# Twelve slots for ranks and list, the first expert named by the last fills, a gather of row 0 ahead, choice behind the tokens

## Chip, core and metric

The kernel runs on one core of a Trainium2 chip. The metric is the device time of one execution in microseconds. The engines are TensorE (PE), VectorE (DVE), ScalarE (ACT), GpSimd (POOL) and SyncE (SP, which issues DMAs).

## What is computed

```python
# linear attention with decay: B 4, H 8, S 768, D 48
state = alpha[t] * state + k[t] (outer) v[t];  y[t] = q[t] @ state
x = y as [3072 tokens, 384]
# first layer: 8 experts of 384 tokens each, F 1024
logits = x @ w_gate                     # [3072, 8]
for idx in argsort(-logits.flatten()):  # highest first
    tok, e = idx // 8, idx % 8
    if assigned[tok] < 0 and counts[e] < 384: assigned[tok] = e; counts[e] += 1
out[mask_e] = relu(x[mask_e] @ w1[e]) @ w2[e]
# second layer, the same weights for all tokens, G 1536
out = (silu(x @ w_gate2) * (x @ w_val)) @ w_out
```

## The kernel before

The attention part works through 24 units (4 batches by 6 chunks of 128 tokens), writes its rows to x_rows in memory and leaves the logits as [128 partitions, 24 tiles, 8 experts]; token t * 128 + p is in tile t, partition p. Its last units overlap the start of the routing.

The greedy assignment is computed in phases: in each, all free tokens choose their best open expert, and a search finds the threshold at which the first expert is full. The first phase has four rounds (first_rounds_vector, first_rounds_tensor). In each, DVE compares every token's best logit with 31 cuts (compare, L809), PE counts by cut and expert (L840), DVE marks the full cuts (find_full, L816 and L817), PE counts those (L844) and DVE raises the base (raise_base, L822). Then `take` (L954 to L968) gives tokens above the base to their experts; PE sums them (ps_room, L1011); DVE finds the newly full expert (L887, L888), marks its tokens (L891, L894), and writes the expert's number to `order` (tell_order, L944 and L946), for which SP waits before it loads that expert's weights. PE ranks the marked tokens within their tile and sums the tiles (L1015 and L1016, 24 columns each). DVE turns the ranks into rows and columns of the list (L900 to L914), builds at_row, one 128 x 128 matrix for each of 24 tiles in two halves (L922), PE multiplies 24 times (L1023), and DVE reduces the sums to slot_token (L928), which has 3 x 128 token numbers. GpSimd gathers the three tiles of rows (gather_first, L1615). PE turns each with three transposes (L1877), ACT and DVE split it in x_high and x_low (L1683, L1686; L1761, L1764), and the first expert's products begin (L1778). While GpSimd gathers, PE runs 20 products of 512 columns that nothing reads (WARM_TURNS, L1871).

Each expert is then computed for its 384 tokens: 8 stages of up and down products with a ring of four weight chunks, 12 stages of gate, value and output products; every product is done in three parts, from a high and a low part of both operands. A group of nine products is one stage of one of these. The seven experts but the last carry the next phase's routing between their stages: `route` puts one step of vector_step and tensor_step behind each stage. Step 10 (s == take + 2) names and marks, step 11 ranks, 12 and 13 build at_row, 14 reduces and settles, 15 chooses. The rank products are issued after stage 2 of the second layer, the list products after stage 5. ACT makes w_high from w_raw, and w_low is made by GpSimd in the loop and by DVE (L1749) for the first four chunks. The choice of the second phase (choose, L980 to L989) stands behind these on DVE and ahead of x_low.

Each link of the routing waits on its own semaphore count for the one before; the order of all work on an engine is the order in which it is written. If a check of the routing fails, an exact routing and a second run of the layers follow.

Of the kernel before, what the change touches and what calls it, by code (L numbers as in the profile page):

```python
# [32 lines left out]
WARM_TURNS = 20  # L33
# [510 lines left out]
SLOTS = 10  # L544

# [4 lines left out]
QUICK_LINKS = 48  # L550
# [5 lines left out]
Operands = namedtuple("Operands", "best is_over got room_now newly_full rank past past_next at_col cols_past row")  # L556
# [14 lines left out]
class QuickRouting:  # L571
# [22 lines left out]
    def __init__(self, nc, ctx, logits, slot_token, order, failed):  # L594
# [3 lines left out]
        def sem(name):  # L598
# [19 lines left out]
        self.cut_tab = sb("cut_tab", [P, ROUNDS, CUTS - 1])  # L618
        self.cuts = sb("cuts", [P, ROUNDS, CUTS - 1])
# [10 lines left out]
        self.place = rest[:, TILES * E:TILES * (E + 1)]  # L630
        self.lows = sb("lows", [P, B, CH - 1])
# [12 lines left out]
        self.mine = sb("mine", [P, TILES], BF16)  # L644
        self.before = sb("before", [P, TILES])
        rank = sb("rank", [P, TILES])
        past = sb("past", [P, TILES, 2 * T3])
        at_col = sb("at_col", [P, TILES, T3])
        cols_past = sb("cols_past", [P, TILES])
        row = sb("row", [P, TILES], BF16)  # L650
        self.token_parts = sb("token_parts", [P, TILES, T3, 2], BF16)
        self.still_free = sb("still_free", [P, TILES], BF16)
        self.first = Operands(self.best, is_over, got, room_now, newly_full, rank, past[:, :, 0:T3], past[:, :, T3:2 * T3], at_col,
                              cols_past, row)
# [5 lines left out]
        self.below = sb("below", [P, P], BF16)  # L660
# [3 lines left out]
        self.col_starts = sb("col_starts", [P, T3 + 1])  # L664
        self.lane = sb("lane", [P, 1])
        self.tiles = sb("tiles", [P, TILES])
# [22 lines left out]
        self.judged = sem("judged")  # L689
        self.at = [0, 0]  # L690


    CONSTS = 5
    SET = 12 + FINE_ROUNDS

    def use(self, bank):
# [4 lines left out]
        self.ps_rank = bank[:, 4 * E:4 * E + 2 * TILES]  # L701
        self.ps_token = bank[:, 4 * E + 2 * TILES:4 * E + 2 * TILES + 2 * T3]
# [5 lines left out]
        def words(count):  # L708
# [9 lines left out]
        past_next, at_col = (shared[:, n * TILES * T3:(n + 1) * TILES * T3].rearrange("p (t c) -> p t c", t=TILES)  # L718
                             for n in range(2))

        assert at[0] > CAP
        best, self.low_apart, self.expert_numbers = (words(count) for count in (TILES, 1, E))
        self.later = Operands(best, self.free, got, room_now, newly_full, self.free, self.first.past, past_next, at_col,
                              self.first.cols_past, self.number)

    def load(self, sp, consts):
        for dst, name in ((self.cut_tab[:, :, :].rearrange("p a b -> p (a b)"), "cuts"),
                          (self.numbers[:], "count"),
                          (self.col_starts[:], "col_starts"), (self.lane[:], "lane"), (self.tiles[:], "tiles")):
            sp.dma_start(dst, consts[name]).then_inc(self.consts_in, 16)  # L730

    def set_up(self, pool):
        for ap, value in ((self.ones, 1.0), (self.ones2, 1.0), (self.assigned, 0.0), (self.free_cap, BIG),
                          (self.room, float(CAP)), (self.room_or_big, float(CAP)),
                          (self.full_before, 0.0), (self.zeros, 0.0), (self.filled, 0.0), (self.odd, 0.0)):
            pool.memset(ap[:], value).then_inc(self.ready, 1)
        for n in range(FINE_ROUNDS):
            pool.memset(self.fine_scale[:, n:n + 1], float(FINE_CUTS) ** -(n + 1)).then_inc(self.ready, 1)

    def set_up_tables(self, pool):  # L740
        pool.wait_ge(self.consts_in, 16 * self.CONSTS)

        pool.tensor_scalar(self.below[:], self.numbers[:], self.lane[:, 0:1], -1.0, ALU.is_lt,
                           ALU.mult).then_inc(self.ready, 1)
# [80 lines left out]
    def first_rounds_vector(self, dve):  # L825
        for n in range(ROUNDS):
            if n > 0:
                self.raise_base(dve, n, self.cuts[:, n - 1, 0:1])
            for i in range(2):
                tiles = slice(i * TILES // 2, (i + 1) * TILES // 2)  # L830
                self.compare(dve, self.best[:, tiles], tiles, self.cuts[:, n, :])
            self.find_full(dve, n + 1, CUTS - 1)
        self.raise_base(dve, ROUNDS, self.cuts[:, ROUNDS - 1, 0:1])

    def first_rounds_tensor(self, pe):
        for n in range(ROUNDS):
            for i in range(2):
                pe.wait_ge(self.over_cut_ready, 2 * n + i + 1)
                for t in range(i * TILES // 2, (i + 1) * TILES // 2):
                    mm = pe.matmul(self.ps_count[0:CUTS - 1, :], self.at_row[:, t, 0:CUTS - 1], self.choice[:, t, :],  # L840
# [3 lines left out]
            pe.matmul(self.ps_full, self.cut_full[0:CUTS - 1, 0:1].broadcast_to([CUTS - 1, P]),  # L844
                      self.ones[0:CUTS - 1, 0:1], start=True, stop=True).then_inc(self.cut_found, 1)
# [5 lines left out]
    def vector_step(self, dve, p, s):  # L851

        link = lambda ins: self.link(dve, ins)
        o = self.operands(p)
# [29 lines left out]
        if s == take + 2:  # L884

            dve.wait_ge(self.got_summed, p + 1)
            link(dve.tensor_tensor(o.room_now[:, :], self.room[:], self.ps_room, ALU.subtract))  # L887
            link(dve.scalar_tensor_tensor(out=o.newly_full[:, :], in0=o.room_now[:, :], scalar=0.5,  # L888
                                          in1=self.full_before[:], op0=ALU.is_lt, op1=ALU.subtract))
            newly_full = o.newly_full[:, :].unsqueeze(1).broadcast_to(te)  # L890
            link(dve.tensor_tensor(self.marks[:], self.assigned[:], newly_full, ALU.mult))  # L891
            if o is self.later:
                self.tell_order(dve, p, o)
            dve.tensor_reduce(self.mine[:], self.marks[:], AX_X, ALU.max).then_inc(self.mine_ready, 1)  # L894
            if o is self.first:
                self.tell_order(dve, p, o)
        if s == take + 3:

            dve.wait_ge(self.mine_ranked, p + 1)
            link(dve.tensor_tensor_scan(self.before[:], self.ps_rank[:, TILES:2 * TILES], self.zeros[:], 0.0,  # L900
                                        ALU.add, ALU.add))
            link(dve.tensor_tensor(o.rank[:, :], self.ps_rank[:, 0:TILES], self.before[:], ALU.add))
            link(dve.tensor_tensor(o.rank[:, :], o.rank[:, :], self.mine[:], ALU.mult))
            tc = [P, TILES, T3]
            for past, c in ((o.past, 0), (o.past_next, 1)):
                link(dve.tensor_tensor(past, o.rank[:, :].unsqueeze(2).broadcast_to(tc),
                                       self.col_starts[:, c:c + T3].unsqueeze(1).broadcast_to(tc), ALU.is_ge))
            link(dve.tensor_tensor(o.at_col[:, :, :], o.past, o.past_next, ALU.subtract))
            link(dve.tensor_tensor(o.cols_past[:, :], o.past[:, :, 1], o.past_next[:, :, 1], ALU.add))
            link(dve.scalar_tensor_tensor(out=o.row[:, :], in0=o.cols_past[:, :], scalar=-float(P),  # L910
                                          in1=o.rank[:, :], op0=ALU.mult, op1=ALU.add))

            link(dve.tensor_scalar(self.token_parts[:, :, :, 0], o.at_col[:, :, :], self.lane[:, 0:1], None, ALU.mult))
# [1076 lines left out]
```

## Time and profile before

| | |
|---|---|
| median of 3 runs | 849.14 us (849.04 to 849.73) |
| profiled execution | 849.57 us, span 847.7 us |
| PE busy | 819.5 us |
| DVE busy | 508.6 us |
| ACT, POOL busy | 299.5, 236.1 us |

Times in the rows are microseconds from the start of the span. A row of the chain gives start, length and what the end of the program was waiting for at that time; a row of a timeline gives start, length, engine, line, operation, tiles and shapes, and in brackets how long the engine had been idle and what ended it.

### The profile page before, as it was taken

Reading aid. Unit: us, or ns where it says so; the run is one execution under the profiler, and the core shown is the slowest. Engines: PE = TensorE matmul, PEld = TensorE weight load, DVE = VectorE, ACT = ScalarE, POOL = GpSimd, SP = SyncE. Lnnn points to the kernel's source line nnn. Section 1 sums busy time; section 2 is a strip of 40 time slices with the busy share of each in tenths; the row PEclk is TensorE's granted clock in tenths of the full one; section 3 lists DMA queues with packets and bytes.
Section 4 is the critical chain, followed back from the end, with each engine's and each line's share of the span. In section 5 each row is a group of like instructions: output and inputs, shape, how many; then the busy total and the mean of one; then the engine's idle time right before and its main releaser. Section 6 shows DMA issues by size and latency. Waiting matters only on the chain.

```text
span 847.7 us, 16569 instructions
## 1 busy us (share of the span) xinstructions
PE 819.5 (97%) x6116; PEld 783.7 (92%) x6116; DVE 508.6 (60%) x1095; ACT 299.5 (35%) x607; POOL 236.1 (28%) x263
## 2 busy tenths in 40 slices
PE   9999993899999999999999999999999999999995
PEld 5889883699999999999999999999999999999995
DVE  9999986846554655465546554665466546642332
ACT  2566652432343224323332333233323332333221
POOL 4222210388613041304130414050405040504001
PEclk9999996899999999999999999999999999999998
DMA  8898852402300230023002300230023002300000
GB/s 294 282 323 290 285 173 73 161 1 75 103 19 9 74 102 19 9 74 102 19 9 74 102 19 9 74 102 19 9 74 102 19 9 74 102 18 11 1 1 32
DMA packets 25858, 70.98 MB, mean 84 GB/s; under 512 B 3808, under 2 KB 10464, under 8 KB 25824
## 3 DMA queue, kind: packets, MB, share of 16 engines
q1 hardware_dynamic: 19296, 56.39, 20.2%
q0 software_dynamic: 3072, 9.44, 3.3%
q10 hardware_dynamic: 3456, 4.72, 1.5%
q8 instruction: 18, 0.29, 0.1%
q14 instruction: 16, 0.13, 0.1%
HBM read 61.10 MB, written 9.44 MB: 83 GB/s over the span
## 4 chain that ended last, share of the span: by engine, by line
PE 81%; DVE 2%; issue 1%; DMA 0%; POOL 0%; POOLq 0%; ACT 0%; ACTq 0%
PE ps_up L1778 48%; PE ps_acc L1778 30%; PE ps_turn_again L1002 1%; PE ps_turn_again L1023 1%; PE ps_turn L1784 1%; PE ps_turn_again L840 0%; DVE quick_at_row L922 0%; DMA x_tok<-x_rows,slot_token 0%; DVE quick_at_row L809 0%; PE ps_up L1784 0%; POOL x_tok L1615 0%; POOLq L1911 0%; DVE quick_base L822 0%; PE ps_turn_again L844 0%; DVE quick_fills L816 0%
## 5 line engine op out<-in xcount | busy, mean ns | idle before, releaser
L1778 PE MATMUL ps_up<-z_high,gated_high 128*128 128x384 f32 x576 | 197.8, 343 | 0.0
L1778 PE MATMUL ps_up<-z_high,gated_low 128*128 128x384 f32 x576 | 194.6, 338 | 0.0
L1778 PE MATMUL ps_up<-z_low,gated_high 128*128 128x384 f32 x576 | 193.6, 336 | 0.0
L1560 POOL TENSOR_TENSOR w_low<-w_raw,w_high 128x384 fp32r<-128x384 f32 x120 | 118.6, 1014 | 248.3 <-ACT w_high L1641 248.0
L1778 PEld LDWEIGHTS ps_up<-z_high,gated_high 128*128 128x128 f32 x576 | 108.3, 188 | 0.0
L1778 PEld LDWEIGHTS ps_up<-z_low,gated_high 128*128 128x128 f32 x576 | 108.1, 188 | 0.2
L1778 PEld LDWEIGHTS ps_up<-z_high,gated_low 128*128 128x128 f32 x576 | 108.3, 188 | 0.0
L1725 DVE TENSOR_TENSOR act_out<-ps_up,act_out 128x384 f32<-128x384 f32 x96 | 53.4, 557 | 89.8 <-ACT act_out L1657 88.1
L1660 ACT CAST u_high<-ps_up 128x384 fp32r<-128x384 f32 x96 | 46.1, 480 | 169.3 <-DVE ps_up L1729 169.3
L1657 ACT ACTIVATE act_out<-ps_up 128x384 f32<-128x384 f32 x96 | 47.2, 492 | 142.0 <-PE ps_up L1778 141.9
L1778 PE MATMUL ps_acc<-gated_high,u_high 128*128 128x384 f32 x288 | 97.4, 338 | 0.0
L1778 PE MATMUL ps_acc<-gated_low,u_high 128*128 128x384 f32 x288 | 96.8, 336 | 0.0
L1778 PE MATMUL ps_acc<-gated_high,u_low 128*128 128x384 f32 x288 | 96.5, 335 | 0.0
L1583 POOL DMA_INDIRECT out<-o_tok,to_rows x24 | 23.6, 985 | 224.5 <-ACT o_tok L1669 189.9
L1732 DVE TENSOR_TENSOR u_low<-ps_up,u_high 128x384 fp32r<-128x384 f32 x96 | 53.6, 558 | 52.4 <-ACT u_high L1660 51.9
L1714 DVE SCALAR_TENSOR_TENSOR h_low<-ps_up,h_high 128x384 fp32r<-128x384 f32 x64 | 35.7, 558 | 71.0 <-ACT h_high L1637 69.2
L1729 DVE TENSOR_TENSOR ps_up<-act_out,ps_up 128x384 f32<-128x384 f32 x96 | 54.0, 562 | 39.5 <-PE ps_up L1778 37.3
L1641 ACT CAST w_high<-w_raw 128x768 fp32r<-128x768 f32 x64 | 53.6, 837 | 47.6 <-PE ps_acc L1778 34.9
L1778 PE MATMUL ps_up<-x_high,w_high 128*128 128x384 f32 x192 | 66.8, 348 | 0.1
L1778 PE MATMUL ps_acc<-h_high,w_high 128*128 128x384 f32 x192 | 64.8, 337 | 0.0
L1778 PE MATMUL ps_up<-x_low,w_high 128*128 128x384 f32 x192 | 64.4, 336 | 0.0
L1778 PE MATMUL ps_up<-x_high,w_low 128*128 128x384 f32 x192 | 64.4, 336 | 0.0
(220 smaller groups left out, 1420.9 us busy)
## 6 DMA issues: line engine op xcount, KB each, us to landing
w_raw<-in_experts SPq DMA_DIRECT2D x64, 384.0 KB, 3.0
qka_in<-in_qka SPq DMA_DIRECT2D x22, 770.5 KB, 5.8
gated_raw<-in_gated SPq DMA_DIRECT2D x12, 576.0 KB, 5.7
v_in<-in_v SPq DMA_DIRECT2D x24, 192.0 KB, 5.0
x_rows<-y_rows ACTq DMA_DIRECT2D x24, 192.0 KB, 3.7
qka_in<-in_qka SPq DMA_DIRECT2D x2, 512.0 KB, 5.1
qka_in<-in_qka SPq DMA_DIRECT2D x2, 258.5 KB, 3.8
out<-o_tok,to_rows POOLq DMA_INDIRECT x24
```

The source lines that it names most:

```text
L1002: mm = pe.matmul(self.ps_count, self.at_row[:, j, :], self.slot_choice[:, j, :], start=(j == 0), stop=(j == SLOTS - 1))
L1023: mm = pe.matmul(self.ps_token, self.at_row[:, t, :], self.token_parts[:, t, :, :].rearrange("p a c -> p (a c)"), start=(t == 0), stop=(t ...
L1560: part = pool.tensor_tensor(w.low[:, m % RING, cols], w.raw[:, m % RING, cols], w.high[:, m % RING, cols].bitcast(F32), ALU.subtract)
L1583: pool.indirect_dma_start(out=out, out_offset=bass.IndirectOffsetOnAxis(ap=to_rows[:, t:t + 1], axis=0), in_=o_tok[:, t, :], in_offset=Non ...
L1641: act.copy(w.high[:, m % RING, :], w.raw[:, m % RING, :]).then_inc(w_high_ready, 1)
L1657: act.activation(act_out[:, j % 2, :], ps_up[j % 2][0][:, 0:CAP], ACT.Sigmoid).then_inc(sigm_ready, 1)
L1660: act.copy(u_high[:, j % 2, :], ps_up[j % 2][0][:, 0:CAP]).then_inc(u_high_ready, 1)
L1714: dve.scalar_tensor_tensor(out=h_low[:, m % 2, :], in0=ps_up[m % 2][0][:, 0:CAP], scalar=0.0, in1=h_high[:, m % 2, :].bitcast(F32), op0=AL ...
L1725: dve.tensor_tensor(act_out[:, j % 2, :], ps_up[j % 2][0][:, 0:CAP], act_out[:, j % 2, :], ALU.mult).then_inc(silu_ready, 1)
L1729: dve.tensor_tensor(ps_up[j % 2][0][:, 0:CAP], act_out[:, j % 2, :], ps_up[j % 2][1][:, 0:CAP], ALU.mult).then_inc(gated_ready, 1)
L1732: dve.tensor_tensor(u_low[:, j % 2, :], ps_up[j % 2][0][:, 0:CAP], u_high[:, j % 2, :].bitcast(F32), ALU.subtract).then_inc(u_low_ready, 1)
L1778: mm = pe.matmul(acc, lhs[a], rhs[b], start=(first and i == 0), stop=(last and i == 2))
```

## The change

The list has 12 slots a partition instead of 24 tiles: a token's slot is its place among the marked tokens of its partition (place_mine), and hold_mine finds the tile of each slot. PE ranks partitions with one product of one column (ahead, mine_count) where it had two of 24, and the list takes 12 products with at_row of 12 x 128. A partition with more than 12 marked tokens sets the failure flag through `most`.

In the first phase the fourth round has 32 cuts, and its fills go as [32, 8] straight to PE, which sums them per expert; the expert with the highest sum is the first. The take, the room and settling come behind the list on DVE (first_settle_vector), and PE's room product behind its list products. GpSimd folds the expert's number to `order` with five small operations (tell_first). Before them it issues one gather of row 0, 128 times, into x_tok. Of the first four w_low, two are made on DVE and two on GpSimd, behind the gathers. The warm products are 6, 4 and 3, ahead of the transposes of the three tiles. choose stands behind x_low. A tensor of 96 words and the changed sizes move the addresses of what is allocated later.

```diff
-WARM_TURNS = 20
+WARM_TURNS = (6, 4, 3)
+LISTED = 12
+SPACER = 96
+FIRST_LOWS = 2
@@ first_rounds_vector, behind the last compare
-            self.find_full(dve, n + 1, CUTS - 1)
-        self.raise_base(dve, ROUNDS, self.cuts[:, ROUNDS - 1, 0:1])
+            if n < ROUNDS - 1:
+                self.find_full(dve, n + 1, CUTS - 1)
+        link(dve.tensor_tensor(self.base_under[:], self.base[:], self.cuts[:, ROUNDS - 1, 1:2], ALU.subtract))
+        dve.wait_ge(self.cuts_counted, ROUNDS)
+        dve.tensor_tensor(self.last_fills[:, :], self.ps_count[0:CUTS, :], self.room_or_big[0:CUTS, :],
+                          ALU.is_ge).then_inc(self.cut_full_ready, 1)
+        dve.wait_ge(self.cut_found, ROUNDS)
+        link(dve.tensor_reduce(self.level[:], self.ps_room, AX_X, ALU.max))
+        dve.tensor_tensor(o.newly_full[:, :], self.ps_room, self.level[:, 0:1].broadcast_to([P, E]),
+                          ALU.is_equal).then_inc(self.first_known, 1)
+        link(dve.scalar_tensor_tensor(out=self.base[:], in0=self.level[:], ...))
+        link(dve.tensor_tensor(self.marks[:], self.choice[:], o.newly_full ...))
+        link(dve.tensor_reduce(self.mine_any[:], self.marks[:], AX_X, ALU.max))
+        link(dve.scalar_tensor_tensor(out=o.mine[:, :], in0=self.best[:], scalar=self.base[:, 0:1], in1=self.mine_any[:],
+                                      op0=ALU.is_ge, op1=ALU.mult))
+    def first_list_vector(self, dve):
+        self.count_mine(dve, o.mine[:, :])
+        self.place_mine(dve, 0, o)
+        self.hold_mine(dve, o)
+        dve.wait_ge(self.mine_ranked, 1)
+        self.rank_mine(dve, o)
+        self.part_tokens(dve, o)
+        for i in range(2):
+            self.find_rows(dve, o, i)
+        self.list_tokens(dve, 0)
+    def tell_first(self, pool):
+        pool.wait_ge(self.first_known, 1)
+        pool.tensor_tensor(self.first_part[:], self.first.newly_full[0:1, :], self.tiles[0:1, 0:E], ALU.mult)...
+        for n, half in enumerate((4, 2, 1)):
+            pool.tensor_tensor(self.first_part[:, 0:half], self.first_part[:, 0:half], self.first_part[:, half:2 * half], ALU.add)...
+        pool.tensor_scalar(self.order[0:1, 0:1], self.first_part[:, 0:1], float(E - 1), None, ALU.min)...
+    def first_settle_vector(self, dve):
+        self.take(dve, 0)
+        self.leave_room(dve, 0, o)
+        self.settle(dve, 0, o)
+    def first_list_tensor(self, pe):
+        self.rank_tensor(pe, 0)
+        self.list_tensor(pe, 0, 1)
+        self.room_tensor(pe, 0)
+    def place_mine(self, dve, p, o):
+        link(dve.tensor_tensor_scan(self.mine_place, o.mine[:, :], self.zeros[:], 0.0, ALU.add, ALU.add))
+        link(dve.tensor_tensor(o.place_of[:, :], self.mine_place, o.mine[:, :], ALU.mult))
+    def hold_mine(self, dve, o):      # by_slot = [P, 12, 24]
+        link(dve.tensor_tensor(self.mine_held, place_of, slot numbers, ALU.is_equal))
+        link(dve.tensor_tensor(self.mine_part, self.mine_held, tile numbers, ALU.mult))
+        link(dve.tensor_reduce(self.slot_tile[:], self.mine_part, AX_X, ALU.add))
+    def rank_mine(self, dve, o):      # five links of 12 elements: slot_rank, rank, past_one, cols_past, row
+    def part_tokens(self, dve, o):    # three links of 36: at_col, token_parts 0, token_parts 1
@@ tensor_step, s == take + 5
-                for t in range(i * TILES // 2, (i + 1) * TILES // 2):
-                    mm = pe.matmul(self.ps_token, self.at_row[:, t, :],
+            for j in range(i * LISTED // 2, (i + 1) * LISTED // 2):
+                mm = pe.matmul(self.ps_token, self.at_row[:, j, :], ...
@@ gather_first
+                pool.indirect_dma_start(
+                    out=x_tok[:, 0, :], out_offset=None, in_=x_rows,
+                    in_offset=bass.IndirectOffsetOnAxis(ap=quick.row_zero[:, 0:1], axis=0)).then_inc(quick.warmed, 16)
+                quick.tell_first(pool)
+                pool.wait_ge(quick.warmed, 16)
                 pool.wait_ge(quick.listed, 1)
                 for t in range(T3):
                     pool.indirect_dma_start(
...
+                for m in range(FIRST_LOWS, RING):
+                    pool.wait_ge(w_low_ready, m)
+                    split_low(0, m)
@@ vector, not again
+                quick.first_rounds_vector(dve)
+                quick.first_list_vector(dve)
+                quick.first_settle_vector(dve)
+                quick.keep_apart(dve)
+                for m in range(FIRST_LOWS):
+                    first_low(m)
                 for t in range(T3 - 1):
                     dve.wait_ge(first_high_ready, t + 1)
...
+                quick.choose(dve)
+                quick.end_first_phase()
@@ tensor, not again
                 quick.first_rounds_tensor(pe)
-                for s in range(quick.TAKE, steps):
-                    route(0, s, False)
-                for n in range(WARM_TURNS):
-                    pe.matmul(ps_up[0][0] ...)
+                quick.first_list_tensor(pe)
                 for t in range(T3):
+                    for n in range(WARM_TURNS[t]):
+                        pe.matmul(ps_up[0][0] ...)
                     pe.wait_ge(first_rows[t], 16)
```

## Rows read from the trace of the kernel before

**Rows 1.** The page, busy time, share and instructions of each engine.
```profile
PE 819.5 (97%) x6116; PEld 783.7 (92%) x6116; DVE 508.6 (60%) x1095; ACT 299.5 (35%) x607; POOL 236.1 (28%) x263
```

**Rows 2.** The chain of waits, 141 to 164 us: start, length, what.
```profile
141.11 0.17 DVE quick_fills L816
...
147.53 3.44 DVE quick_at_row L922 x2
...
151.54 0.18 DVE slot_token L928
...
156.45 3.04 DMA x_tok<-x_rows,slot_token
...
159.53 0.34 PE ps_acc L1877
...
160.21 3.39 PE ps_up L1778 x18
163.60 1.56 PE ps_acc L1778 x9
```

**Rows 3.** The timeline of DVE, 142 to 165 us.
```profile
142.64 0.49 DVE L959 TENSOR_REDUCE quick_got_rows<-quick_got 128x8 bf16<-128x192 bf16 x1
...
143.74 0.17 DVE L888 SCALAR_TENSOR_TENSOR quick_newly_full<-quick_room_now,quick_full_before 128x8 f32<-128x8 f32 x1
143.94 0.36 DVE L891 TENSOR_TENSOR quick_marks<-quick_assigned,quick_newly_full 128x192 bf16<-128x192 bf16 x1
...
152.62 3.56 DVE L1749 TENSOR_TENSOR w_low<-w_raw,w_high 128x768 fp32r<-128x768 f32 x4
...
156.50 0.35 DVE L980 TENSOR_TENSOR quick_limited<-logits,ps_turn_again 128x192 f32<-128x192 f32 x1
...
158.84 0.16 DVE L989 COPY quick_base<-ps_turn_again 128x1 f32<-128x1 f32 x1
...
160.40 0.48 DVE L1764 TENSOR_TENSOR x_low<-ps_up,x_high 128x128 fp32r<-128x128 f32 x2
...
163.76 0.41 DVE L864 TENSOR_TENSOR quick_at_row<-ps_turn_again,quick_numbers 128x240 f32<-128x240 f32 x1
```

**Rows 4.** The timeline of PE, 151 to 164 us.
```profile
151.36 6.87 PE L1871 MATMUL ps_up<-quick_idt 128*128 128x512 bf16 x20
158.06 0.82 PE L1877 MATMUL ps_acc<-quick_idt,x_tok 128*128 128x128 f32 x6
...
163.79 0.33 PE L1778 MATMUL ps_acc<-h_low,w_high 128*128 128x384 f32 x1
```

**Rows 5.** POOL: the first gathers, a copy, and all gathers of the loop (min/median/max).
```profile
152.69 1.94 POOL L1615 DMA_INDIRECT x_tok<-x_rows,slot_token  x1 [35.44 <-DVE slot_token L928]
154.93 1.21 POOL L1615 DMA_INDIRECT x_tok<-x_rows,slot_token  x1 [0.30 <-issue]
...
219.85 0.18 POOL L1547 COPY from_rows<-slot_token 128x3 uint32<-128x3 uint32 x1 [0.28 <-DVE slot_token L928]
...
L1552 POOL DMA_INDIRECT x_tok<-x_rows,from_rows x21: 942/957/1007, 220.8 to 735.9; - x21
```

**Rows 6.** Windows: length, busy of PE, PEld, DVE, ACT, POOL, granted clock, DMA.
```profile
132.00:134.00 2.00, 1.14 (x25) 0.89 (x25) 1.15 (x4) 1.89 (x2) 0.00 (x0) 0.58 0.24 68
...
156.00:156.25 0.25, 0.25 (x2) 0.15 (x1) 0.25 (x2) 0.00 (x0) 0.15 (x1) 0.54 0.44 172
```

**Rows 7.** The chain of waits in the loop's first turn, 288 to 305 us.
```profile
288.12 1.56 PE ps_acc L1778 x9
289.69 0.03 PE ps_turn_again L1015
...
304.00 0.60 PE ps_turn_again L1023 x24
304.60 3.26 PE ps_up L1778 x18
```

**Rows 8.** The timeline of ACT, the first cast of the first expert's weights.
```profile
149.31 1.78 ACT L1641 CAST w_high<-w_raw 128x768 fp32r<-128x768 f32 x2 [11.38 <-DMA w_raw<-in_experts]
```

More of the change, by code:

```diff
@@ L555 @@
 Programs = namedtuple("Programs", "sync gpsimd scalar vector tensor")
-Operands = namedtuple("Operands", "best is_over got room_now newly_full rank past past_next at_col cols_past row")
+Operands = namedtuple("Operands", "best is_over got room_now newly_full mine place_of rank row at_col")
 def has_failed(eng, quick):
@@ L643, in __init__ @@
         self.marks = sb("marks", te, BF16)
[L644 to L654, printed above, removed]
+        self.mine_count = sb("mine_count", [P, 1], BF16)
+        self.most = sb("most", [P, PHASES + 1])
+        self.mine_any = sb("mine_any", [P, TILES])
+        mine = sb("mine", [P, TILES])
+        place_of = sb("place_of", [P, TILES])
+        self.slot_tile = sb("slot_tile", [P, LISTED])
+        self.slot_rank = sb("slot_rank", [P, LISTED])
+        self.past_one = sb("past_one", [P, LISTED])
+        self.cols_past = sb("cols_past", [P, LISTED])
+        rank = sb("rank", [P, LISTED])
+        row = sb("row", [P, LISTED], BF16)
+        at_col = sb("at_col", [P, LISTED, T3])
+        self.token_parts = sb("token_parts", [P, LISTED, T3, 2], BF16)
+        self.still_free = sb("still_free", [P, TILES + PHASES + 1], BF16)
+        self.any_wrong = sb("any_wrong", [P, 1], BF16)
+        self.first = Operands(self.best, is_over, got, room_now, newly_full, mine, place_of, rank, row, at_col)
         self.odd = sb("odd", [P, 3])
@@ L843, in first_rounds_tensor @@
             pe.wait_ge(self.cut_full_ready, n + 1)
[L844 to L845 removed]
+            if last:
+                mm = pe.matmul(self.ps_room, self.ones[0:CUTS, :], self.last_fills[:, :], start=True, stop=True)
+            else:
+                mm = pe.matmul(self.ps_full, self.cut_full[0:CUTS - 1, 0:1].broadcast_to([CUTS - 1, P]),
+                               self.ones[0:CUTS - 1, 0:1], start=True, stop=True)
@@ L853, in vector_step @@
         link = lambda ins: self.link(dve, ins)
-        o = self.operands(p)
+        o = self.later
         te = [P, TILES, E]
@@ L892, in vector_step @@
[L892 to L896, printed above, removed]
+            link(dve.tensor_tensor(self.marks[:], self.assigned[:],
+                                   o.newly_full[:, :].unsqueeze(1).broadcast_to(te), ALU.mult))
+            self.tell_order(dve, p, o)
+            link(dve.tensor_reduce(o.mine[:, :], self.marks[:], AX_X, ALU.max))
@@ L897, in vector_step @@
+            self.place_mine(dve, p, o)
+            self.count_mine(dve, o.mine[:, :])
         if s == take + 3:
             dve.wait_ge(self.mine_ranked, p + 1)
[L900 to L911, printed above, removed]
@@ L925, in vector_step @@
[L925 to L938 removed]
+            self.hold_mine(dve, o)
@@ L939, in vector_step @@
+            self.rank_mine(dve, o)
+        if s == take + 4:
+            self.part_tokens(dve, o)
+        if s in (take + 4, take + 5):
+            self.find_rows(dve, o, s - take - 4)
+        if s == take + 6:
+            self.list_tokens(dve, p)
+            self.settle(dve, p, o)
         if s == take + 7:
@@ L1740, in expert, with first_low @@
                 dve.tensor_copy(o_tok[:, T3 - 1, :], ps_acc[T3 - 1][:, 0:DM]).then_inc(last_o_copied, 1)
-            if not again:
-                quick.first_rounds_vector(dve)
-                quick.take(dve, 0)
-                for s in range(quick.TAKE + 1, steps - 1):
-                    route(0, s, False)
-            for m in range(RING):
+            def first_low(m):
                 dve.wait_ge(w_high_ready, m + 1)
@@ L1750, in vector @@
                                   ALU.subtract).then_inc(w_low_ready, 1)
-            if not again:
-                quick.keep_apart(dve)
-                quick.choose(dve)
-                quick.end_first_phase()
             if again:
+                for m in range(RING):
+                    first_low(m)
                 for k in range(K1):
```

197 lines of the change are left out of this document (130 added, 67 removed).

## The prediction

> **What bounds the kernel now.** I read the page's engine totals first: PE is busy for 97% of the span [rows 1]. Then the chain of waits in order of time. After the attention part it leaves PE and runs mostly through DVE until 151.7 us, then through GpSimd and its gathers to 159.5, and from 160.21 on it is PE without a break until the tail [rows 2]. From there to the end each PE microsecond taken out is one off the time, and DVE or GpSimd work counts only if PE waits for it. Ahead of 160.21 it is the other way round: DVE's links count, and PE only with what it does after the list. So the sum has two parts: the entry (when the first expert's first product starts) and the seven later routing phases, as they stand in PE's queue.
>
> **The list of the first expert.** I take start-to-start times on DVE as the price of a link: about 0.20 us for 24 elements or fewer (L888 at 143.74, L891 at 143.94), 0.39 for 192 and 0.44 for 240 (a busy time of 0.36 and 0.41 and 0.03 to the next; [rows 3]). From the end of the last L816 at 141.28 to the start of the token reduction at 151.54 are 10.26 us [rows 2]. After the change the same stretch is: PE's 32-row product as L844's, 0.27 with its hand-overs; level, newly_full and base 0.62; marks and mine_any 0.78; mine, count, scan, place 0.84; three operations on 12 x 24 = 288 elements, which the trace does not have: not under the 240-element link (0.44) and not over it in proportion (0.44 x 1.2 = 0.53), taken 0.49, 1.47 together; five links of rank_mine 1.00; three of part_tokens on 36 elements, between 0.20 and 0.39, near the small one, 0.23 each, 0.69; at_row with 768 instead of 1536 elements per half, (1.72 - 0.12) / 2 + 0.12, about 0.89, twice, 1.78; the last six products instead of twelve 0.32. Sum 7.77, so 2.5 us earlier: the reduction starts at about 149.1. Gone from the path are cut_full, the take (0.27 + 0.39 + 0.49 + 0.39) and leave_room, which come later on DVE. The rank product is issued after count_mine and hides behind scan, place and hold (2 us against 0.25). The bounds of this step are 2.1 to 2.8.
>
> **The gathers.** Before, the first issue took 1.94 us and the second 1.21; the 21 of the loop take 0.957 in the middle, 1.007 at most [rows 5]. If the extra is that of a first use, the gather of row 0 pays it around 135 us, when GpSimd has nothing else and stores have landed, and the real ones save 0.94 + 0.26 = 1.2 us. If they save nothing it is 0; the row of the loop is the nearest for a second use, so 1.2. Third issue then at about 152.65, and with its 3.04 us to landing [rows 2] the last rows are there at 155.7 instead of 159.49; the first at 153.1, the second at 154.4.
>
> Beside the two long issues DVE ran L1749, whose operands are both in SBUF; the third, from 156.45, lay beside choose [rows 2, 3, 5]. The Trainium skill (SBUF — State Buffer, "SBUF: two separate sides") says that a VectorE operation with two SBUF inputs and a GpSimd operation that reads SBUF take one shared port by turns, each for a whole instruction. By that rule the excess comes from the neighbour, not from first use; the third issue would then lie beside the moved first_low and take up to 1.94 again, its rows landing at 156.7. The trace can't tell the two apart; it only shows that L1749 itself was not slowed. That is a rival below.
>
> **PE up to the first product.** PE's queue holds the room product between list and warm turns, and it waits for the take: list at 149.1, then 0.2 and 1.15 for is_over, got, got_rows [rows 3], so 150.5. The turns therefore start at 150.55, against 151.36 before [rows 4]. The granted clock fell to 0.50 in 132 to 134 and went back to 1.00 at 156.2 [rows 6], so 1.2 GHz until then, 2.4 after; PE had been busy without a gap for 4.87 us when it rose. A turn is 0.427 at 1.2 GHz (the twenty: 4.87 / 0.427 = 11.4 of them, then 8.6 x 0.216). Now: six turns to 153.1; three transposes at twice the 0.11 pitch of [rows 4] to 153.8; four turns to 155.5; the clock, if it again takes 4.87 us from 150.55, rises at 155.4; three transposes 0.33, three turns 0.65, to 156.45; last transposes and cast as before 0.68 (159.53 to 160.21), first product at 157.1. That is 3.1 us earlier than 160.21. Two ends: a clock that is up by 154.5 leaves only the rows, 155.7 + 0.68 = 156.4, 3.8 earlier; one that isn't up at all gives 158.4, 1.8 earlier, with what then follows in the rival. So of the 3.7 us by which list and gather move, about 0.6 goes to turns put between the transposes.
>
> **What is late next.** (a) choose (L980 to L989, 2.5 us [rows 3]) now stands behind x_low. x_low ended 0.67 us after the first product; then choose to +3.2, h_low to +3.8. PE took h_low's first product at 163.79, 3.58 after 160.21 [rows 2, 4]. So a wait of 0.2 us, 0 to 0.5; the next h_low has over a microsecond of room. (b) Weights: DVE does take, leave_room, settle and keep_apart from 149.3 to about 152.7, then two w_low at 0.89 each to 154.4, before PE needs them. The other two, by GpSimd, take 2 us each, behind the third issue and w_low 1, to 156.4 and 158.4; PE needs them 5 and 8 us after 157.1. Without that room each would cost its lateness. Casts of w_high began at 149.31 [rows 8], soon enough even if the first order came no earlier. (c) The five small GpSimd operations that tell SP the expert: the copy of 3 numbers took 0.18 [rows 5], so 0.9 to 1.5 in all from 141.95; even 3 us would put the order no later than before, where it came after the whole take, and by (b) no cast would be late. GpSimd's queue behind them holds only the gather, which waits for 149.3 anyway. (d) Two memsets more, one table load less and lane_part lie in GpSimd's idle time in attention, 0.1 us at worst.
>
> **The seven later phases.** PE's list products fall from 24 to 12: 0.60 us for 24 [rows 7], so 0.30 a phase; of the two rank products (0.03 and 0.02) one goes, 0.03. 7 x 0.33 = 2.3 us, all on the path, bounds 2.0 to 2.5. DVE gets 0.6 us more in step 10 and about the same in step 11 (2.5 against 2.5), and less in 12 and 13. PE has no wait for DVE in this stretch now: it runs on after the 24 products into the next stage [rows 7], and the longest step now, choose with 2.5 us, is hidden in stages 4.8 us long (from the rank products at 289.69 to the list products at 304.00 are three). So nothing.
>
> **Sum.** -3.1 + 0.2 - 2.3 = -5.2 us. The profiled execution took 849.57 (span 847.7 and 1.9 around it), which is 0.43 over the median of 849.14. From the first the sum gives 844.4, from the second 843.9; I say 844.1.
>
> **Rivals.**
> 1. The clock stays low past the first product. For it: in the new entry PE's work is cut by waits and turns, and short bursts of 1 us or so from 133 to 149 raised nothing. If it takes 4.87 us from the first product at 158.4, the products up to then lose half, 2.4 us: the entry is 0.6 later than before plus 0.2, the phases give 2.3, so 847.7. If it rises at 158, 845.4. Against: the turns begin earlier than before and join with gaps near 0.
> 2. The port, as above: a third issue of up to 1.94 instead of 0.957 puts the last rows at 156.7, the first product at 157.4: 844.4 from the median, and with a first issue of 1.94 too 845.3. What speaks for it is that both long issues lay beside L1749.
> 3. Slower: other addresses. All big operands move in SBUF. PE spends 1.56 us on nine products (173.6 ns each, more than 384 columns at 2.4 GHz need), and the kernel has 468 x 8 = 3744 of them. From 1.4 ns a product (0.8%) this eats the 5.2 us; at 1% it is 6.5 us and the time 850.4. Against: the products of h with the ring's weights at 163.60 [rows 2] and of the gated weights with u at 288.12 [rows 7] come from quite different places and both take 1.56 for nine.
> 4. It doesn't do what it says: were more than 12 tokens of an expert in one partition, the list would be short and the kernel would route and compute again, eight stretches of 85 us more. Counting the reference's own assignment, no partition has more than 9.
>
> **Chances.** The forecast's own course (842.9 to 845.1) 0.62; rivals 1 and 2 beyond that (845.1 to 847.7) 0.26; rival 3 0.11 (0.07 slower, 0.03 within 0.2%, 0.01 still faster); rival 4 0.01. The far end of rival 1 is within 0.2% too, 0.01. Of a measurement of this kernel about 0.2%, 1.7 us, can be told from no change. Faster 0.88, same 0.04, slower 0.08. The range is 842.7 to 846.9: below, everything at its good end (3.8, 0 wait, 2.5: 842.8); above, most of rival 1.
>
> **What would show it.** The first expert's token reduction near 149.1; three issues of about 1.0, 0.95, 0.95; the clock's rise before 157; the first product at 156.4 to 158.4; one PE wait of about 0.2 us for h_low; 0.30 for the list products of each phase; the nine-product groups still 1.56. It is wrong if the loop groups differ from 1.56, if a PE wait recurs in each phase, or if the rise comes after the first product.

## The result, and the profile after

The changed kernel takes 841.19 us (median of 4 runs, 840.79 to 841.45); the kernel before took 849.28 beside it. The ratio is 0.9902 with a 95% interval of 0.9890 to 0.9914: faster by 8.1 us, where I forecast 5.2 and a time of 844.1. The direction was right, the size was not, and the time lies below the range (842.7 to 846.9). The profiled execution took 841.45.

The page after, answering to [rows 1]:

```profile
span 839.5 us, 16444 instructions
...
PE 811.9 (97%) x6005; PEld 776.7 (93%) x6005; DVE 505.7 (60%) x1134; ACT 299.8 (36%) x607; POOL 242.9 (29%) x276
```

PE is 7.6 us less busy. Eight lists at 0.30 less are 2.4, and the warm turns (6.87 before, 2.72 + 1.91 + 0.81 after) are 1.4 less; the other half must come from products that both kernels have. The chain of waits of the kernel after over the entry, answering to [rows 2] (start, length, what):

```profile
141.23 0.17 DVE quick_last_fills L862
...
147.17 1.84 DVE quick_at_row L980 x2
...
149.42 0.17 DVE slot_token L987
...
150.39 3.19 DMA x_tok<-x_rows,slot_token
...
157.66 0.67 DVE x_low L1903 x3
158.34 0.27 DVE quick_limited L1106
...
160.59 0.17 DVE quick_base L1115
160.98 0.57 DVE h_low L1853
161.59 1.51 PE ps_acc L1919 x7
```

The list reduction starts at 149.42 (forecast 149.1), and h_low has become a link of the chain, behind choose, as forecast. PE's timeline, answering to [rows 4], has the first product at 157.67 (forecast 157.1), and in brackets the idle time ahead of h_low's first product:

```profile
150.75 2.72 PE L2012 MATMUL ps_up<-quick_idt 128*128 128x512 bf16 x6
...
157.67 0.44 PE L1919 MATMUL ps_up<-x_high,w_high 128*128 128x384 f32 x1
...
161.59 0.44 PE L1919 MATMUL ps_acc<-h_low,w_high 128*128 128x384 f32 x1 [0.16 <-DVE h_low L1853]
```

GpSimd's timeline, answering to [rows 5]. The third issue takes 1.64:

```profile
133.69 1.19 POOL L1744 DMA_INDIRECT x_tok<-x_rows,quick_row_zero  x1 [16.43 <-DMA x_rows<-y_rows]
...
143.34 0.23 POOL L900 TENSOR_SCALAR order<-quick_first_part 1x1 int32<-1x1 f32 x1
...
150.39 1.06 POOL L1751 DMA_INDIRECT x_tok<-x_rows,slot_token  x1 [6.82 <-DVE slot_token L987]
151.75 0.95 POOL L1751 DMA_INDIRECT x_tok<-x_rows,slot_token  x1 [0.30 <-issue]
153.01 1.64 POOL L1751 DMA_INDIRECT x_tok<-x_rows,slot_token  x1 [0.30 <-issue]
```

Entry and phases together can't give 8.1. The rest is found by holding the same point of two turns of the loop side by side, the count products of choose, which stand behind the same stage in each. The chain of the kernel before, then of the kernel after:

```profile
245.68 3.13 PE ps_up L1778 x18
...
256.61 0.25 PE ps_turn_again L1002 x10
...
294.56 3.16 PE ps_up L1778 x18
...
341.81 0.25 PE ps_turn_again L1002 x10
```

```profile
253.73 0.25 PE ps_turn_again L1128 x10
...
289.87 1.56 PE ps_acc L1919 x9
291.43 3.12 PE ps_up L1919 x18
...
300.80 0.30 PE ps_turn_again L1154 x12
...
338.14 0.25 PE ps_turn_again L1128 x10
```

A turn takes 341.81 - 256.61 = 85.20 before and 338.14 - 253.73 = 84.41 after, 0.79 less, of which list and rank explain 0.33. The rest is in the groups of eighteen: the gate and value products of one stage take 3.12 us instead of 3.16. Twelve such stages in a turn make 12 x 0.04 = 0.48. The nine-product groups stay at 1.56. So the eighteen had been running at 1.58 for nine, and I had compared only the nines. The row at 245.68 is a group of eighteen of the other kind, up products of x with the ring's weights: of the same shape and in the same execution, they take 3.13.

### The profile page after: what moved, and what is told of

Read it like the earlier page. It is cut to its first block, busy times and chain, and to the rows that moved or that the text cites. A ratio compares the mean times of both kernels' runs of the same rounds, so it can differ in the third digit from the quotient of the medians.

```text
span 839.5 us, 16444 instructions
## 1 busy us (share of the span) xinstructions
PE 811.9 (97%) x6005; PEld 776.7 (93%) x6005; DVE 505.7 (60%) x1134; ACT 299.8 (36%) x607; POOL 242.9 (29%) x276
## 4 chain that ended last, share of the span: by engine, by line
PE 81%; DVE 2%; issue 1%; DMA 0%; POOLq 0%; ACT 0%; POOL 0%; DVEq 0%; ACTq 0%
PE ps_up L1919 48%; PE ps_acc L1919 30%; PE ps_turn_again L1128 1%; PE ps_turn L1925 1%; PE ps_turn_again L917 0%; DMA x_tok<-x_rows,slot_token 0%; DVE quick_at_row L831 0%; PE ps_turn_again L1154 0%; PE ps_up L1925 0%; DVE quick_at_row L980 0%; PE ps_up L2012 0%; POOLq L2051 0%; PE ps_acc L2017 0%; DVE quick_base L844 0%; DVE x_low L1903 0%
## 5 line engine op out<-in xcount | busy, mean ns | idle before, releaser
L1919 PE MATMUL ps_up<-z_high,gated_high 128*128 128x384 f32 x576 | 195.7, 340 | 0.0
L1691 POOL TENSOR_TENSOR w_low<-w_raw,w_high 128x384 fp32r<-128x384 f32 x124 | 122.3, 1013 | 243.6 <-ACT w_high L1780 243.1
L1919 PE MATMUL ps_up<-z_high,gated_low 128*128 128x384 f32 x576 | 192.5, 334 | 0.0
L1919 PE MATMUL ps_acc<-h_low,w_high 128*128 128x384 f32 x192 | 64.4, 336 | 0.2 <-DVE h_low L1853 0.2
```

Of the source, the lines that this page charges most:

```text
L1691: part = pool.tensor_tensor(w.low[:, m % RING, cols], w.raw[:, m % RING, cols], w.high[:, m % RING, cols].bitcast(F32), ALU.subtract)
L1919: mm = pe.matmul(acc, lhs[a], rhs[b], start=(first and i == 0), stop=(last and i == 2))
```

## The experiments

All medians are in us. "Before" is the kernel before, run beside it on the same chip.

| kernel | median | before | ratio (95%) |
|---|---|---|---|
| e1_before_all32 | 845.92 | 849.42 | 0.9955 (0.9940 to 0.9969) |
| e2_after_back32 | 845.39 | 849.42 | 0.9952 (0.9935 to 0.9968) |
| e4_before_z32 | 848.94 | 849.42 | 0.9998 (0.9989 to 1.0008) |
| e3_after_no_row0 | 840.33 | 849.42 | 0.9892 (0.9875 to 0.9908) |
| e5_before_all32_z64 | 846.67 | 849.38 | 0.9961 (0.9947 to 0.9975) |
| e7_before_all64 | 849.66 | 849.38 | 1.0004 (0.9994 to 1.0013) |
| e8_before_gated_high32_all64 | 845.92 | 849.38 | 0.9953 (0.9936 to 0.9970) |
| e9_no_row0_choose_split | 840.15 | 849.38 | 0.9886 (0.9869 to 0.9902) |
| e10_after_no_turns | 842.63 | 849.30 | 0.9918 (0.9901 to 0.9934) |
| e11_after_turns_631 | 841.06 | 849.30 | 0.9900 (0.9883 to 0.9916) |
| e12_before_choose_first | 849.19 | 849.30 | 0.9999 (0.9989 to 1.0008) |
| e13_no_row0_split_631 | 840.19 | 849.30 | 0.9889 (0.9872 to 0.9905) |

### The addresses

In the kernel before, the tensors of the layers lie at byte addresses (in a partition) with rest 0 by 64 (what is left over when the address is divided by 64), all but gated_high, which is allocated earlier and has rest 32. The change moves all the others by 32 more than a multiple of 64: they have rest 32 too. (I reckoned the addresses from the sizes of all that is allocated, each start rounded up to 32 bytes; no trace shows them.) The first pair makes this move alone, in each direction.

```diff
 e1, before, behind the tensors of the routing
+        sb("pad", [P, 8])
 e2, after
-SPACER = 96
+SPACER = 88
```

> The kernel before with 8 words of unused memory ahead of all that the layers allocate: gated_low, the ring, x, h, z, u, act_out and the rest lie exactly where the changed kernel has them, nothing else changes. Theory A (the addresses made the products of z with the gated weights shorter, 3.12 instead of 3.16 us for eighteen, some 3.7 us in all): 845.5 us, eighteen products in 3.12, first product still at 160.2. Rival B (the new routing steps in the phases, with other DVE and GpSimd work beside PE, made the products shorter): 849.2, 3.16. Rival C (the trace's 0.04 is noise of one execution): 849.2.

> The changed kernel with its spacer of 88 words instead of 96: all layer tensors lie where the kernel before has them. Theory A: 3.7 us longer than the changed kernel, 844.9 us, eighteen products of z in 3.16. This would be the time of the change without its addresses, and is near the 844.1 that was forecast. Rivals B and C: 841.2, 3.12.

Padding alone, with no other change, takes 849.42 - 845.92 = 3.5 us off the kernel before; taking the move back costs the kernel after 845.39 - 841.19 = 4.2. A group of eighteen in the chain of e1, then a group of e2:

```profile
295.47 3.12 PE ps_up L1779 x18
```

```profile
193.02 3.17 PE ps_up L1919 x18
```

96 stages (8 experts by 12) times 0.04 is 3.8, between the two. This part of the gain is shown from both sides, though e1's median is uncertain by some tenths: its five runs lie at 845.34 to 845.92 and at 846.88 and 846.95, and the profiled one, 846.95, lost time to a clock that fell (last section). What is left open is which operand's place does it. e4 moves z and all behind it, and so leaves gated_low where it was; e5 moves all and z and u back to rest 0; e7 moves by 64 instead of 32; e8 moves gated_high too, to rest 0.

```diff
 e4, before, ahead of z_high
+        sb("pad_z", [P, 8])
 e5: the pads of e1 and e4
 e7: the pad of e1 with 16 words
 e8: the pad of e1, and ahead of gated_high
+        sb("pad_g", [P, 8], F32)
```

> The kernel before with 8 unused words right ahead of z_high: z, u, act_out, o_tok move by 32 bytes; gated_low, the ring, x and h stay. If A holds and it is the place of the streamed operand z by itself, or of z against gated_high, that counts: 845.5, like all moved. If it is the place of gated_low (the stationary operand, against gated_high), 849.2.

> The kernel before with 8 unused words ahead of gated_low and 8 more ahead of z_high: gated_low, the ring, x and h are at +32 bytes, z, u, act_out, o_tok at +64. Moving everything by 32 gave 845.9, moving z and what follows by 32 alone gave 848.9. Theory G (only gated_low's place against gated_high's counts): 845.9 again. Theory R (stationary and streamed operand must leave the same rest when the address is divided by 64; gated_high lies at 32, z would be back at 0): slow again, 849.

> The kernel before with 16 unused words ahead of gated_low: all that the layers allocate moves by 64 bytes, so every rest by 64 is as before. Theory R: 849.4, eighteen products of z in 3.16. If any other place than the old one would do: 845.9.

> The kernel before with 8 unused words ahead of gated_high and 8 ahead of gated_low: gated_high moves from a rest of 32 to one of 0, the layers' tensors move by 64 and keep their rest of 0, so weights and streamed operands have one rest, 0, where the fast kernels have 32. Theory R: 845.9, 3.12. If the layers' own rest of 32 is what counts: 849.4, 3.16.

The chains of e5, e7 and e8, one fence each (e4 has 3.15 for its group at 294.48):

```profile
294.10 3.12 PE ps_up L1780 x18
297.21 1.58 PE ps_acc L1780 x9
```

```profile
294.79 3.17 PE ps_up L1779 x18
```

```profile
294.58 3.12 PE ps_up L1780 x18
```

The column "turn" is one turn of the loop, from one of its count products to the same one a turn later.

| kernel | gated_high, gated_low, z by 64 | eighteen | turn | time |
|---|---|---|---|---|
| before | 32, 0, 0 | 3.16 | 85.20 | 849.3 |
| e7 | 32, 0, 0 (all 64 on) | 3.17 | 85.21 | 849.66 |
| e4 | 32, 0, 32 | 3.15 | 85.13 | 848.94 |
| e5 | 32, 32, 0 | 3.12 | 84.87 | 846.67 |
| e1 | 32, 32, 32 | 3.12 | 84.75 | 845.92 |
| e8 | 0, 0, 0 | 3.12 | 84.70 | 845.92 |

The eighteen are slow when gated_high and gated_low have unlike rests and fast when they have the same, 32 or 0. The turns of the loop say the same, and the clock of the entry has no part in them. A move of 64 does nothing, one of z alone 0.01 a group. In this group PE loads them in turn (high, low, high for the three parts of a product) and streams z; the up and down products load w_high and w_low in turn, which have like rests in both kernels and took 1.56 for nine in both. e8 rules out that 32 is simply the better rest. e5 rules out the other rule on trial, that the loaded and the streamed operand must agree: z is at 0 and the gated weights at 32, and the eighteen take 3.12. Whether 64 is the number that counts is not shown: where the two have like rests by 64 here, they have like rests by 128 and by 256 too. A second, smaller effect is in e5: u at 0 with both gated weights at 32 lengthens the group of nine with u (1.58), and e5 takes 0.75 us more than e1. In that group PE loads u and streams the gated weights. I have no rule for that one, since with gated_high at 32, gated_low at 0 and u at 0 (before) this group takes 1.56. Why the engine's loads or reads care for the rest, no run here shows.

### The gather of row 0 and the third issue

```diff
 e3, after, gather_first
-                pool.indirect_dma_start(
-                    out=x_tok[:, 0, :], out_offset=None, in_=x_rows,
-                    in_offset=bass.IndirectOffsetOnAxis(ap=quick.row_zero[:, 0:1], axis=0)).then_inc(quick.warmed, 16)
...
-                pool.wait_ge(quick.warmed, 16)
```

> The changed kernel without the gather of row 0. If the long first issues of before (1.94 and 1.21 us) were a first use of the gather, as the forecast had it: first issue again about 1.9, second 1.2, the rows 1.2 us later, first product at about 158.6 instead of 157.67, time 842.0. If they were the port shared with L1749 on DVE, whose operands are both in memory: first and second issue stay at 1.0 to 1.2 beside the small DVE operations, third 1.64 beside the two w_low as now, time 841.2 to 841.4.

GpSimd, DVE and PE of e3, from three timelines:

```profile
149.75 1.30 POOL L1747 DMA_INDIRECT x_tok<-x_rows,slot_token  x1 [6.33 <-DVE slot_token L987]
151.36 0.96 POOL L1747 DMA_INDIRECT x_tok<-x_rows,slot_token  x1 [0.31 <-issue]
152.63 0.95 POOL L1747 DMA_INDIRECT x_tok<-x_rows,slot_token  x1 [0.30 <-ACT w_high L1776]
...
152.74 1.83 DVE L1879 TENSOR_TENSOR w_low<-w_raw,w_high 128x768 fp32r<-128x768 f32 x2
...
156.72 0.45 PE L1915 MATMUL ps_up<-x_high,w_high 128*128 128x384 f32 x1
```

Neither course that I expected came: without the gather of row 0 the kernel is faster still, 841.19 to 840.33, and the first product moves from 157.67 to 156.72. The list reduction starts at 149.28 here and the first issue 0.47 behind it; with row 0 gathered it starts 0.97 behind (149.42, 150.39), while its own length falls only from 1.30 to 1.06. So the row-0 gather, with the wait for it, costs 0.26 net on the first issue, and through that start another 0.69 on the third. What sets this delay is open: in the kernel before, with no gather ahead, the first issue comes 1.15 behind the start of the reduction (151.54, 152.69). The kernel after has w_low beginning at 152.87, ahead of the third issue:

```profile
152.87 1.82 DVE L1883 TENSOR_TENSOR w_low<-w_raw,w_high 128x768 fp32r<-128x768 f32 x2
```

It starts 0.14 before the issue (153.01, 1.64 long). In e3 the issue is first by 0.11 and takes 0.95 (e9 and e13 likewise). e2, whose third issue is again behind its w_low, shows the same price (e10 and e11 too, 1.65 and 1.64):

```profile
152.93 1.65 POOL L1751 DMA_INDIRECT x_tok<-x_rows,slot_token  x1 [0.30 <-ACT w_high L1780]
```

The reverse test is on the kernel before: take w_low away from beside the issues, leave the first use.

```diff
 e12, before, vector
+            if not again:
+                quick.keep_apart(dve)
+                quick.choose(dve)
+                quick.end_first_phase()
             for m in range(RING):
                 dve.wait_ge(w_high_ready, m + 1)
                 dve.tensor_tensor(w.low[:, m, :], ...)
-            if not again:
-                quick.keep_apart(dve)
-                quick.choose(dve)
-                quick.end_first_phase()
```

> The kernel before with keep_apart and choose ahead of the four w_low (L1749) instead of behind them. Port theory (the gather's issue is long where it starts beside a DVE operation with both operands in memory): the first two issues, now beside settle and choose, take 1.0 to 1.3 and 0.95 us instead of 1.94 and 1.21, and one that starts during a w_low takes 1.2 to 1.9. First-use theory: 1.94 and 1.21 as before. The w_low end at about 159.1, so the time may stay near 849.

The gathers and w_low of e12:

```profile
152.66 1.17 POOL L1615 DMA_INDIRECT x_tok<-x_rows,slot_token  x1 [35.45 <-DVE slot_token L928]
154.14 0.96 POOL L1615 DMA_INDIRECT x_tok<-x_rows,slot_token  x1 [0.30 <-issue]
155.40 0.95 POOL L1615 DMA_INDIRECT x_tok<-x_rows,slot_token  x1 [0.30 <-issue]
...
155.54 3.56 DVE L1753 TENSOR_TENSOR w_low<-w_raw,w_high 128x768 fp32r<-128x768 f32 x4
```

The issues of 1.94 and 1.21 in [rows 5] become 1.17 and 0.96: most of the excess was the neighbour. The 0.22 that are left (0.35 in e3) may be a first use or the small DVE operations beside it; no run parts the two. Each w_low lasts 0.95 by its own record in the kernels before and after. In the kernel after the one that was under way at the third issue's start ends at 153.83, and the issue ends 0.82 behind it (154.65); in the kernel before, at the second issue, the two ends are 155.32 and 156.14, 0.82 apart. So, as far as these two rows show, the issue waits for the end of that operation and is not held by the next. This agrees with the port rule of the Trainium skill (SBUF — State Buffer, "SBUF: two separate sides"), by which the operation that starts first has the shared port for the whole instruction. The other half of the rule, that whatever comes second is blocked, the traces don't bear out for DVE: in e3 and e12 w_low starts second, within the third issue, and lasts 0.95 all the same. The time of e12 is no other (849.19): its rows come earlier, but the twenty turns start at 151.48 and hold PE until 158.35, and DVE's x_low, now behind the four w_low, keeps PE's next products until 160.50.

### The wait for h_low and the turns

e9 is e3 with the first four operations of choose between the x_low of tile 0 and of tile 1; e13 is e9 with WARM_TURNS (6, 3, 1); e11 and e10 change only the turns of the kernel after.

```diff
 e9 and e13, without row 0, vector, in the loop over tiles
+                    if t == 0:
+                        quick.choose(dve, both=False)
...
-                quick.choose(dve)
+                quick.choose_cuts(dve)
 e11 and e13
-WARM_TURNS = (6, 4, 3)
+WARM_TURNS = (6, 3, 1)
 e10
+WARM_TURNS = (0, 0, 0)
```

> The changed kernel without the gather of row 0 (840.33) and with the first four links of choose put between the first two x_low, where DVE waited for ACT for 0.9 to 1.5 us; the last four stay behind x_low. Theory: the wait for the first h_low goes (PE's first product of h_low at 3.6 instead of 3.9 us after the first product), 0.3 us: 840.0. Rival: the four links, 1.3 us, delay the second x_low instead and with it the first product, since DVE's gap was 0.88 us without the row-0 gather: 840.3 to 840.7.

> The changed kernel without the gather of row 0, with choose split around the second x_low, and 6, 3 and 1 warm products: what the runs so far point to. If the turns between the transposes still cost: 839.6. If the rows or DVE bound it: 840.1, as without the shorter turns.

> The changed kernel with 6, 3 and 1 warm products instead of 6, 4 and 3. If the three last transposes are late because of the turns between (the first product at 157.67, the rows at about 156.1), the first product comes 0.5 to 0.9 us earlier and the time is 840.5. If the third rows bound it, 841.0 to 841.2.

> The changed kernel without any of its 13 warm products. The transposes then start when the rows land, so the first product at about 156.9 instead of 157.67, in PE time that is at 1.2 GHz. The forecast's reckoning (the clock rises 4.9 us after PE begins to be busy without a gap, whenever that is): rise at about 161.8, the products up to then at half speed, 2.4 us lost, 842.8 us in all. Rival (the rise comes at a time that the program's start sets, about 155 to 157 us, if only PE is then busy; it was 156.1 to 156.3 in both first traces, with the turns starting 0.6 us apart): here PE is idle before the rows, so the rise comes at the next such time, 158.5 to 163: 841.5 to 843.5. Neither expects less than 841.2.

PE's first product and the first of h_low in e9:

```profile
157.09 0.44 PE L1924 MATMUL ps_up<-x_high,w_high 128*128 128x384 f32 x1
...
160.69 0.33 PE L1924 MATMUL ps_acc<-h_low,w_high 128*128 128x384 f32 x1
```

160.69 - 157.09 = 3.60, as in the kernel before (3.58), so the wait is gone; but the first product is 0.37 later than in e3, because the second x_low is (156.59 against 156.16). 840.15 against 840.33 is within the spread of the two (839.89 to 840.66). e13, with fewer turns, is at 840.19: its first product comes at 156.67, but then PE waits 0.19 for x_low. e11 (841.06) equals the kernel after (841.19): its third tile of rows comes no earlier, and PE stands idle for it 1.22 us. Its timeline:

```profile
156.99 0.33 PE L2017 MATMUL ps_acc<-quick_idt,x_tok 128*128 128x128 f32 x1 [1.22 <-DMA x_tok<-x_rows,slot_token]
```

So in the kernel after the rows are as late as the turns; taking turns away gains nothing while the third issue is blocked. Without any turns (e10) the first product comes at the same time (157.72) and the clock later. Windows of e10 (length, busy of PE, PEld, DVE, ACT, POOL, granted clock, DMA):

```profile
158.00:160.00 2.00, 2.00 (x7) 2.00 (x8) 1.83 (x8) 1.37 (x2) 0.81 (x1) 0.50 0.91 277
160.00:161.00 1.00, 1.00 (x5) 1.00 (x4) 0.76 (x3) 0.00 (x0) 0.00 (x0) 0.50 0.98 283
161.00:161.25 0.25, 0.25 (x2) 0.25 (x2) 0.00 (x0) 0.25 (x1) 0.00 (x0) 0.50 1.23 283
161.25:161.50 0.25, 0.25 (x3) 0.25 (x2) 0.00 (x0) 0.24 (x1) 0.00 (x0) 1.00 0.64 258
```

The clock is 0.50 until 161.25 and 1.00 behind it, so 3.5 us of products run at half speed. That is 1.8 us lost, less the 0.3 for h_low, which is then hidden: 1.5, and 842.63 - 841.19 = 1.44 is what the thirteen turns are worth.

## Why the prediction was wrong

**The sum.** Of the 8.1 us, 2.2 come from the entry (the first product of h_low moved from 163.79 to 161.59), 2.3 from the phases (7 x 0.33) and 3.5 to 4.2 from the addresses. Without the addresses the kernel (e2) stands 4.0 below the kernel before, where I had said 5.2. The miss is thus the address term, which I had at zero, less an entry of 2.2 instead of 2.9. With 3.5 for the addresses the terms add to 8.0, with 4.2 to 8.7. The time of e2, 845.39, lies in the range that I gave.

**Rival 3, the addresses.** This is the step that failed. I priced a change of place only as a loss ("slower: other addresses") and set it against two groups of nine, the one with h at 163.60 and the one with u at 288.12, "both take 1.56 for nine" [rows 2, 7]. The first loads w_high and w_low in turn, whose rests are alike; the second loads u and streams the gated weights. Neither loads the two gated tensors in turn. The group that does, eighteen products, stood at 3.16 in the same chain (294.56, shown above), which is 1.58 for nine: the loss was already there and visible. Had I divided that row by two, the rival would have had a gain as its likelier side: 96 x (3.16 - 2 x 1.56) = 3.8 us. "It is wrong if the loop groups differ from 1.56" was a test of the nines alone, and they stayed at 1.56.

**The list of the first expert.** 8.02 us from the end of the last fills (141.40) to the reduction (149.42) against 7.77: mis-sized by 0.25. at_row took 0.92 each instead of 0.89; the small links of base, mine and token_parts 0.25 to 0.29 instead of about 0.20 to 0.23.

**The gathers.** I took the excess of the first issues as that of a first use, and gave the port the second place. It was mostly the neighbour on DVE: e12 and e3 show it. Row 0 was to save 1.2 and costs 0.9 (e3). The rival's own numbers (rows at 156.7, first product 157.4) are the nearest of all to what happened (157.67); its time of 844.4 is 0.2 too much if it is added to the median (843.9 + 0.3). That the first product lay within my bounds of 156.4 to 158.4 is in part luck, since this term had the wrong sign.

**PE up to the first product.** The turns started at 150.75 (forecast 150.55), but the clock rose at 156.1, not at 155.4. Windows of the kernel after:

```profile
155.75:156.00 0.25, 0.25 (x2) 0.08 (x1) 0.00 (x0) 0.00 (x0) 0.25 (x2) 0.50 0.73 283
156.00:156.25 0.25, 0.25 (x3) 0.22 (x2) 0.00 (x0) 0.00 (x0) 0.25 (x1) 0.81 0.49 191
```

That is the time of [rows 6], though the turns began 0.6 earlier. The 4.87 us are no constant: e11, with the same first six turns, rose at 153.6:

```profile
153.50:153.75 0.25, 0.10 (x1) 0.00 (x0) 0.25 (x1) 0.00 (x0) 0.25 (x1) 0.86 1.12 203
```

e1 and e8, with the entry of the kernel before (turns from 151.44 and 151.78, there 151.36), rose at 154.1 and 157.3, where it rose at 156.2. The Trainium skill (TensorE: Matmul & The Clock Gate, "What's actually happening") says that the point of the transition varies by half a microsecond either way, with where the first matmul happens to fall. The rows agree that it varies, but by about three microseconds between e1 and e8, and I should have given the clock a range instead of a time. Here it cost little, since the rows bound the start as well.

**What is late next.** Right: one wait of PE for h_low. The timeline shows 0.16 idle; from first product to h_low it is 3.92 us against 3.58, so 0.3, within the forecast's 0 to 0.5. No cast and no w_low was late, and GpSimd's five operations for the expert end at 143.57, long before anything waits for them.

**The phases.** Right: the list takes 0.30 (300.80, x12) instead of 0.60, and PE waits for nothing in the turn that I read (250 to 345).

**Rivals 1 and 4.** The clock was up before the first product, and the quick path held, so neither happened. e10 shows rival 1's price: with the rise 3.5 us behind the first product the kernel still takes 842.63. Rival 1's 847.7 has the phases too, but not the addresses, and has the first product at 158.4 instead of 157.72 and the rise 4.87 behind it.

## What to carry to other kernels

Before costing a change that shifts allocations, divide every group of the same product shape by its count: if one group is slower than the others per product, a place costs something already, and a shift can give it back as well as take more. A warm-up or an early gather is to be measured by what it does to the start of the next one, not only by its length. Where two engines share a resource, ask which one starts first at the new times: 0.1 us of order decided 0.7 us here.

The best version is the kernel after without its gather of row 0 (840.2 to 840.3 in three forms: e3, e9, e13).

## What the runs showed of the hardware

- Products of 384 columns run 1% slower (3.16 against 3.12 us for eighteen) when the two weights that PE loads in turn have unlike address rests by 64 bytes (32 and 0; whether 64, 128 or 256 is the number that counts is open); the kernel has 96 such groups, and 32 bytes of padding per partition give 3.5 us of 849.
- An indirect DMA issue takes 0.95 us, 1.64 when a w_low with two SBUF inputs has started 0.14 before it, and 0.95 when the issue starts 0.11 ahead. The first gather of a program takes 0.2 to 0.35 more (1.17 and 1.30 beside small DVE operations).
- With an earlier gather and the wait for it the next issue starts later (0.97 against 0.47 us from the start of the list reduction); the kernel before, without either, has 1.15. Why, no run shows.
- The clock can fall again behind the first product. In the profiled execution of e1, which took 846.95 where its median is 845.92, it rose at 154.1 and fell to 0.50 from 161.0 to about 164.3, while PE was busy throughout. Before that PE had been idle for half of 158 to 160, waiting for rows, but never for a whole microsecond:

```profile
158.00:160.00 2.00, 1.01 (x6) 0.62 (x6) 1.86 (x6) 0.66 (x3) 0.00 (x0) 1.00 0.34 98
160.00:162.00 2.00, 1.86 (x8) 1.75 (x8) 0.82 (x4) 1.79 (x4) 0.00 (x0) 0.74 0.62 207
162.00:164.00 2.00, 2.00 (x8) 2.00 (x8) 0.59 (x2) 0.49 (x1) 0.00 (x0) 0.50 0.95 252
```
